# Dividing two vector-engine pairs around the first Fourier transform of a fused attention and two-MLP kernel

## The chip, the cores and the metric

The kernel runs on one core of a Trainium2 chip. The metric is the device time of one execution in microseconds (us), lower is better. The engines are TensorE (PE in the profile; PEld is its weight loading), VectorE (DVE), ScalarE (ACT), GpSimd (POOL) and SyncE (SP, which here only issues transfers). They run side by side and wait for each other on semaphores.

## The reference

Everything is float32. Attention has batch 4, 8 heads, 576 tokens and head width 64; only the 32 largest scores of a row are kept:

```python
scores = q @ k.T / sqrt(64)
kth = np.partition(scores, -32, axis=-1)[..., -32:-31]
attn = softmax(np.where(scores >= kth, scores, -1e9)) ; x = attn @ v      # x: (4, 576, 512)
mixed = real(fft(fft(x, axis=1), axis=2)) ; u = x + mixed                 # first block
u = u + relu(layernorm(u) @ w_ch1) @ w_ch2                                # 512 -> 2048 -> 512
out = u + relu(layernorm(u) * g_ln @ v_ch1) @ v_ch2                       # second block, own weights
```

## The kernel before

**Tiles and slots.** The scores are cut into 144 tiles of 128 rows by 576 columns (NT = 36 for each batch). The loop of each engine goes over "slots" s; in slot s, TensorE transposes the probabilities of tile s (`probs_T`, L684), makes the scores of tile s+4 (`scores`, L636/L642), multiplies the probabilities of a finished pair of tiles with the values (`values`, L700/L706) and transposes the result back (`values_back`, L715). ScalarE empties PSUM behind it: `probs_out` (L927), `scores_out` (L886), `x_out`, `x_back` (L951, which puts the rows of x into U and counts s_x_sb), and it computes the exponentials (`exps`, L915 and L920).

**Pairs on VectorE.** `pair(n)` handles tiles 2n and 2n+1. It has four rounds; each takes the 8 largest of both tiles (L1140, twice) and, except in the last, strikes them out (L1146, twice). Then a masking instruction for each tile (L1153) makes the final probabilities. Pair 17 is the last one of batch 0; pair 18 (tiles 36, 37) and pair 19 (tiles 38, 39) are the two at the "first seam".

**The later scores.** The scores of the last 72 tiles are made early, two tiles at a time: `scores_ahead(e)` (L663/L669) for e = 0 to 35 on TensorE into all four PSUM banks called Big, in slot e+1; `scores_aside(e)` (L897) on ScalarE copies them out in slot e+2, and `store_aside(e)` (L901) sends them to HBM. Each `scores_ahead` waits for the copy of the one before.

**The first seam.** When batch 0's attention is done, VectorE divides its rows by the sums of the softmax and forms sums and differences of mirrored rows and columns (`normal_x`, `pair_x`, `fold_x`, L1162 to L1206). From that TensorE makes the two-dimensional transform in ten "pieces" (`dft_piece`; 0 to 3 at L779/L786 along the tokens, 4 to 9 at L791/L796 along the width), which ScalarE copies out (`piece_out`, L958). They are made in slot SEAM = 37 and use the banks of Big, so the first waits for the copy of the last scores ahead (s_ah_sb) as well as for the folds (s_fold). `combine(0, j)` on VectorE (L1217 to L1228) adds pieces 4+2j and 5+2j to U, `own_stats` takes the layer norm's statistics (L1232, L1236), `normalise` (L1258) scales two blocks of rows, TensorE transposes them (`un_T`, L811), ScalarE and VectorE split them into a high and a low part (L976 and `first_low`, L1264), and the first MLP can start.

**The burst.** In slot START[0] = 39 seven units of the MLP (`mlp1` L735, `mlp2` L752) are made at once on TensorE; from then on there is one unit (at times two) in every slot.

The order on VectorE before: pair 18, then `normal_x(0)`, `pair_x(0)`, `fold_x(0)`; pair 19; then `combined(0, 0)` (combine and statistics), `combine(0, 1)`, the two `normalise(0, j)`, `own_stats(0, 1)`, the two `first_low(j)`, `combined(0, 2)`; pair 20.

Of the kernel before, what the change touches and what calls it, by code (L numbers as in the profile page):

```python
# [14 lines left out]
NT = NHP * TPP  # L15
# [22 lines left out]
WFS = 3  # L38
AHEAD = NT
ASIDE = 4  # L40
KEPT = TILES - 2 * AHEAD
SIDE = (B // 2) * NHP

# [2 lines left out]
BURST = 7  # L46
GROUPS = len(ORDER)
NUNITS = GROUPS * KF
SEAM = NT + 1
FIRST = NT + 3  # L50
SCORED = {4: FIRST + 1, 5: FIRST + 2}
DOUBLE = (45, 52, 59, 66, 71, 82, 87, 96, 101, 105, 111, 121, 126, 132, 138)
# [14 lines left out]
def slot_of(n):  # L67

    return SLOT_OF[n]
# [15 lines left out]
def closing_at(s):  # L85

    if s == START[0]:
        return []
    return [n for n in range(NUNITS) if slot_of(n) == s - 1][-1:]


def turn_slot(t):
# [46 lines left out]
def rstd_slot(p):  # L139

    if ready_pair(p) >= PAIRS:
        return START[p] - 10
    return SEAM + 1 if p == 0 else 2 * (ready_pair(p) - 1)


def width(c):
# [71 lines left out]
def build(nc, q, k, v, g2, w_raw, seq_t, wid_t, alt_t, w_low, sc_ahead, out):  # L218
# [4 lines left out]
    with ctx:  # L223
# [398 lines left out]
        def _(pe):  # L622
# [203 lines left out]
            for s in range(SLOTS):  # L826
                pieces = [(b, i) for b in range(B) for i in range(PIECES) if piece_slot(b, i) == s]
                units = units_at(s)
                if s < TILES:
                    if turns_at(s - 1):  # L830
                        pe.wait_ge(s_unT_sb, last_turn(s))
                    probs_T(s)
                    if s + RING < KEPT and s not in SCORED.values():
                        if last_piece(s) > last_piece(s - 1) > 0 or last_piece(s) == PIECES and s == SEAM + 1:
                            pe.wait_ge(s_pc_sb, last_piece(s))
                        scores(s + RING)
                for n in second_at(s - 1):
                    mlp2(n - 1)
                if s == START[0]:
                    for t in turns_at(s):  # L840
                        un_T(t)
                if s != START[0]:
                    for n in units:
                        if n not in second_at(s):
                            mlp1(n)
                    for t in turns_at(s):
                        un_T(t)
                if s != SEAM and pieces:
                    dft_piece(*pieces[0])
                if s < TILES:  # L850
                    values(s)
                for n in closing_at(s):
                    mlp2(n)
                if s != SEAM and pieces:
                    dft_piece(*pieces[1])
                if s < TILES:
                    values_back(s)
                for n in second_at(s):
                    mlp1(n)
                if 0 < s <= AHEAD:  # L860
                    scores_ahead(s - 1)
                if s == SEAM:
                    pe.wait_ge(s_tab, 48)
                    for b, i in pieces:
                        dft_piece(b, i)
                if s == START[0]:
                    for n in units:
                        mlp1(n)
                        if n > 0:
                            mlp2(n - 1)  # L870
                        if n in SCORED:
                            scores(SCORED[n] + RING)

        @block.scalar
        def _(act):
# [163 lines left out]
            for s in range(SLOTS):  # L1039
                pieces = [(b, i) for b in range(B) for i in range(PIECES) if piece_slot(b, i) == s]  # L1040
                if s < TILES:
                    probs_out(s)
                    if s == START[0]:
                        for t in turns_at(s):
                            un_out(t)
                    if 0 <= s - 2 < AHEAD:
                        scores_aside(s - 2)
                    if s + RING < KEPT:
                        if s not in SCORED.values():
                            scores_out(s + RING)  # L1050
                    elif s % 2 == 0 and s + RING < TILES:
                        scores_in((s + RING) // 2)
                    if s % 2 == 0 and s < 2 * KF:
                        weights_high(s + 1)
                    if 0 <= s - 2 < AHEAD:
                        store_aside(s - 2)
                    if s % 2 == 0 and s + 2 < TILES and s not in (START[0] - 3, START[0] - 1, START[0] + 1) and not late_exps(s):
                        exps(s + 2)
                        exps(s + 3)
                    if s % 2 == 1 and late_exps(s - 1):  # L1060
                        exps(s + 1)
                        exps(s + 2)
                if s != START[0]:
                    for n in units_at(s):
                        if n in second_at(s):
                            continue
                        relu_out(n)
                        if n >= UP:
                            w2_high(n)
                    for t in turns_at(s):  # L1070
                        un_out(t)
                if s != SEAM and pieces:
                    piece_out(*pieces[0])
                if s < TILES:
                    x_out(s)
                if s != START[0]:
                    for n in units_at(s):
                        if n not in second_at(s):
                            highs(n)
                for n in closing_at(s):  # L1080
                    if n % KF == KF - 1 and n < NUNITS - 1:
                        y_out(n // KF)
                if s != SEAM and pieces:
                    piece_out(*pieces[1])
                if s < TILES:
                    x_back(s)
                for n in second_at(s):
                    relu_out(n)
                    highs(n)
                for p in range(GROUPS):  # L1090
                    for j in range(SIZE[p]):
                        if scaled_by_act(p) and s == scale_slot(p, j):
                            normalise(p, j)
                if s % 2 == 1 and s + 1 < 2 * KF:
                    weights_high(s + 1)
                if s == SEAM:
                    exps(s + 1)
                    exps(s + 2)
                    for b, i in pieces:
                        piece_out(b, i)  # L1100
                        if i == 0:
                            high_1(0)
                        if i == 1:
                            high_2(0)
                            high_1(1)
                        if i == 2:
                            high_2(1)
                        if i == 3:
                            high_1(2)
                if s == START[0]:  # L1110
                    for n in units_at(s):
                        relu_out(n)
                        if n > 0:
                            highs(n)
                        if n in (1, 5):
                            exps(s + n // 2 + 1)
                            exps(s + n // 2 + 2)
                        if n in SCORED:
                            scores_out(SCORED[n] + RING)
                for n in units_at(s):  # L1120
                    if UP <= n + 2 < NUNITS:
                        w1_high(n + 2)

        @block.vector
        def _(dve):
            def pair(n):
# [3 lines left out]
                for r in range(ROUNDS):  # L1130
# [12 lines left out]
                    for a, s in enumerate(tiles):  # L1143
                        dve.wait_ge(s_top, t0 + 2 * r + a + 1)
                        src = sc[:, s % RING, :] if r == 0 else wk[:, a, :]
                        nc.vector.match_replace(out=wk[:, a, :], in_to_replace=top[:, s % RING, r, :], in_values=src,  # L1146
                                                imm_value=STRUCK).then_inc(s_struck, 1)
                for a, s in enumerate(tiles):
                    dve.wait_ge(s_exp, s + 1)
                    dve.wait_ge(s_top, t0 + 2 * (ROUNDS - 1) + a + 1)  # L1150
# [94 lines left out]
            def combined(b, j):  # L1245
                combine(b, j)
                own_stats(b, j)
# [47 lines left out]
            dve.wait_ge(s_init, 2)  # L1295
            for n in range(PAIRS):
                pair(n)
                if n == NT // 2:
                    normal_x(0)
                    pair_x(0)  # L1300
                    fold_x(0)
                if n == NT // 2 + 1:
                    combined(0, 0)
                    combine(0, 1)
                    for j in range(SIZE[0]):
                        normalise(0, j)
                    own_stats(0, 1)
                    for j in range(SIZE[0]):
                        first_low(j)
                    combined(0, 2)  # L1310
# [76 lines left out]
```

## Time and profile before

| | |
|---|---|
| three executions | 1359.71, 1361.39, 1363.40 us; median 1361.39 |
| the profiled execution | 1362.1 us in all; its span from first to last instruction 1360.3 us |
| busy share of the span | PE 92%, DVE 81%, ACT 59%, POOL 26% |
| mean granted TensorE clock | 0.977 of full speed |

All rows are from the profiled execution and count from the start of its span. A busy share is an average over the kernel; what matters for this change is the stretch from about 205 to 315 us, around the first seam.

### The profile page before, as it was taken

To read this page: it belongs to the slowest core of one execution; us is meant where nothing else is said; L and a number is where in the kernel's file an instruction comes from. 1 tells how busy PE (TensorE), PEld (TensorE's weight loads), DVE (VectorE), ACT (ScalarE), POOL (GpSimd) and SP (SyncE) were. 2 spreads that over 40 slices of the span, in tenths; PEclk is the share of its full clock that TensorE was granted. 3 is DMA by queue.
4 is the path that set the end of the run, shared out by engine and by line. 5 is a ranking of instruction groups with operands and counts; after the bars stand their busy time and mean duration, and the time that the engine had idled before them with its cause. 6 is when DMAs were issued, how large, how long until landed. Compare 5 with 4: busy or idle time off the path is not lost.

```text
span 1360.3 us, 22775 instructions
## 1 busy us (share of the span) xinstructions
PE 1252.0 (92%) x7944; PEld 1024.3 (75%) x7944; DVE 1101.4 (81%) x2196; ACT 798.4 (59%) x1586; POOL 356.6 (26%) x327
## 2 busy tenths in 40 slices
PE   5776778999999899999988999999989999999999
PEld 3444444787777778788876888887679999999997
DVE  7999999899999989999999779975484454646453
ACT  4777765578777646776665557664353434343442
POOL 2444430122232431223335123333030111212110
PEclk9989978999999899999999999999999999999999
DMA  7899993567757757777885577753244343333342
GB/s 249 321 338 340 327 325 145 186 223 252 244 194 259 236 189 251 267 259 241 263 285 197 168 231 238 259 195 129 80 153 142 123 148 117 128 115 127 119 148 85
DMA packets 118259, 282.21 MB, mean 207 GB/s; under 512 B 29825, under 2 KB 29826, under 8 KB 118146
## 3 DMA queue, kind: packets, MB, share of 16 engines
q1 hardware_dynamic: 106386, 233.55, 51.7%
q10 hardware_dynamic: 10368, 42.47, 8.3%
q0 software_dynamic: 1392, 4.73, 1.1%
q8 instruction: 65, 1.06, 0.3%
q14 instruction: 48, 0.39, 0.1%
HBM read 237.44 MB, written 42.73 MB: 206 GB/s over the span
## 4 chain that ended last, share of the span: by engine, by line
PE 57%; DVE 36%; issue 5%; ACT 1%; POOL 1%; DMA 1%; SPq 0%; ACTq 0%; DVEq 0%
PE Big L752 23%; DVE top L1140 15%; PE Big L735 15%; DVE wk L1146 14%; PE Sp L735 7%; DVE ex L1153 3%; PE Tp L684 3%; PE Sp L779 2%; PE Tp L706 2%; PE Sp L791 1%; DVE st L1232 1%; PE Tp L811 1%; PE Big L779 1%; PE Sp L642 1%; PE Big L791 0%
## 5 line engine op out<-in xcount | busy, mean ns | idle before, releaser
L752 PE MATMUL Big<-wr,hh 128*128 128x512 f32 x1152 | 361.4, 395 | 0.0
L735 PE MATMUL Big<-uh,wr 128*128 128x256 f32 (+1 forms) x1400 | 320.9, 319 | 7.1 <-ACT hh L990 6.8
L1140 DVE MAX8 top<-wk 128x8 f32<-128x576 f32 x432 | 304.3, 745 | 0.0
L735 PEld LDWEIGHTS Big<-uh,wr 128*128 128x128 f32 x1400 | 236.5, 191 | 26.3 <-issue 16.5
L752 PEld LDWEIGHTS Big<-wr,hh 128*128 128x128 f32 x1152 | 217.6, 189 | 41.1
L752 PE MATMUL Big<-wr,hl 128*128 128x512 f32 x576 | 238.7, 414 | 4.8 <-DVE wr L1285 4.6
L512 POOL TENSOR_TENSOR hl<-hf,hh 128x256 fp32r<-128x256 f32 (+1 forms) x126 | 108.5, 861 | 452.5 <-ACT hh L990 452.5
L735 PE MATMUL Big<-ul,wr 128*128 128x256 f32 (+1 forms) x700 | 218.6, 312 | 0.0
L1146 DVE MATCH_REPLACE8 wk<-top,wk 128x576 f32<-128x576 f32 x288 | 211.4, 741 | 0.0
L684 PE MATMUL Tp<-ident,ex 128*128 128x128 f32 x720 | 117.1, 289 | 47.2 <-DVE ex L1153 38.3
L927 ACT ACTIVATE pT<-Tp 128x640 f32<-128x640 f32 x144 | 101.1, 702 | 88.1 <-PE Tp L684 87.9
L684 PEld LDWEIGHTS Tp<-ident,ex 128*128 128x128 f32 x720 | 86.5, 146 | 87.6 <-issue 50.8
L990 ACT ACTIVATE hh<-Big 128x384 fp32r<-128x384 f32 (+1 forms) x175 | 75.5, 432 | 118.1 <-PE Big L735 118.1
L1153 DVE SCALAR_TENSOR_TENSOR ex<-sc,top,ex 128x576 f32<-128x576 f32 x144 | 124.6, 902 | 18.8 <-ACT ex L920 18.7
L752 PEld LDWEIGHTS Big<-wr,hl 128*128 128x128 f32 x576 | 108.5, 188 | 34.8 <-issue 15.7
L735 PEld LDWEIGHTS Big<-ul,wr 128*128 128x128 f32 x700 | 133.5, 191 | 0.0
L1140 DVE MAX8 top<-sc 128x8 f32<-128x576 f32 x144 | 101.6, 746 | 16.6 <-ACT sc L886 9.5
L1146 DVE MATCH_REPLACE8 wk<-top,sc 128x576 f32<-128x576 f32 x144 | 105.7, 741 | 0.0
L920 ACT ACTIVATE ex<-sc,nmx 128x576 f32<-128x576 f32 x144 | 104.0, 769 | 2.3
L506 POOL TENSOR_TENSOR wr<-wf,wr 128x1024 fp32r<-128x1024 f32 x32 | 75.3, 2368 | 111.3 <-DVE top L1140 109.3
L989 ACT ACTIVATE hf<-Big 128x256 f32<-128x256 f32 (+1 forms) x126 | 52.2, 414 | 82.0 <-PE Big L735 82.0
L706 PE MATMUL Tp<-pT,vn 128*64 128x128 f32 x1280 | 87.9, 286 | 12.4 <-ACT pT L927 11.9
(136 smaller groups left out, 1832.1 us busy)
## 6 DMA issues: line engine op xcount, KB each, us to landing
wf<-in_weights SPq DMA_DIRECT2D x208, 512.0 KB, 3.6
wr<-w_low SPq DMA_DIRECT2D x252, 256.0 KB, 4.3
sc<-in_weights SPq DMA_DIRECT2D x48, 512.0 KB, 3.2
sc<-sc_ahead ACTq DMA_DIRECT2D x36, 576.0 KB, 5.6
w_low<-wr SPq DMA_DIRECT2D x32, 512.0 KB, 6.6
sc_ahead<-U ACTq DMA_DIRECT2D x18, 576.0 KB, 5.2
sc_ahead<-un ACTq DMA_DIRECT2D x9, 576.0 KB, 4.1
sc_ahead<-yb ACTq DMA_DIRECT2D x9, 576.0 KB, 6.5
```

The costliest lines, as they stand in the source:

```text
L506: pool.tensor_tensor(wr[:, r, :, 1, :], wf[:, j % WFS, :, :], wr[:, r, :, 0, :].bitcast(f32), ALU.subtract).then_inc(s_wlow, 1)
L512: pool.tensor_tensor(hl[:, n % 2, 0:w], hf[:, n % 2, 0:w], hh[:, n % 2, 0:w].bitcast(f32), ALU.subtract).then_inc(s_hl[0], 1)
L684: last = nc.tensor.transpose(Tp[:, c * P:(c + 1) * P], ex[:, s % RING, c * P:(c + 1) * P], ident[:, :])
L706: last = nc.tensor.matmul(OT[h * D:(h + 1) * D, :], vn[:, par, c, h, 0:D], pT[:, h, c * P:(c + 1) * P], start=(c == 0), stop=(c == C - 1))
L735: last = nc.tensor.matmul(hidden(n), a[:, kd * P:(kd + 1) * P], x[:, kd, 0:P * SIZE[p]], start=(kd == 0 and j == 0), stop=(kd == KD - 1 an ...
L752: last = nc.tensor.matmul(Ac[:, j, :], a[:, n % 2, j * P:(j + 1) * P], w, start=(f == 0 and m == 0), stop=(f == KF - 1 and m == 2))
L920: nc.scalar.activation(ex[:, s % RING, 0:S], sc[:, s % RING, :], ACT.Exp, bias=nmx[:, s % RING:s % RING + 1], scale=1.0 / np.sqrt(D)).then ...
L927: nc.scalar.activation(pT[:, s % 2, :], Tp[:, 0:C * P], ACT.Copy).then_inc(s_pT_sb, 1)
L990: nc.scalar.activation(hh[:, n % 2, 0:w], hidden(n), ACT.Relu).then_inc(s_h_sb, 1)
L1140: nc.vector.max(top[:, s % RING, r, :], src).then_inc(s_top, 1)
L1146: nc.vector.match_replace(out=wk[:, a, :], in_to_replace=top[:, s % RING, r, :], in_values=src, imm_value=STRUCK).then_inc(s_struck, 1)
L1153: nc.vector.scalar_tensor_tensor(out=ex[:, s % RING, 0:S], in0=sc[:, s % RING, :], scalar=top[:, s % RING, ROUNDS - 1, 7:8], in1=ex[:, s % ...
```

## The change

Three things move. On VectorE, `normal_x(0)`, `pair_x(0)` and `fold_x(0)` are issued inside pair 18, behind its second strike-out, and `combined(0, 0)` inside pair 19, behind its third; the two `normalise(0, j)` go ahead of `combine(0, 1)`. On TensorE and ScalarE the ten pieces move from slot 37 to slot 35, and so stand ahead of the transposes of tiles 36 and 37. So that Big is free there, `scores_ahead(0..32)` stay in slots 1 to 33, and 33, 34, 35 are made in slot 35 behind tile 35's values, ahead of the pieces; the copies and stores of 0 to 31 stay, the one of 32 goes to the end of slot 33, and those of 33, 34, 35 to the end of slot 35. The exponentials of tiles 38 and 39 follow the copy of piece 2.

```diff
+LAST = AHEAD - 1
-SEAM = NT + 1
+SEAM = NT - 1
...
+def made_at(s):
+    if s == LAST:
+        return [LAST - 2, LAST - 1, LAST]
+    return [s - 1] if 0 < s < LAST - 1 else []
+def taken_behind(s):
+    return {LAST - 2: [LAST - 3], LAST: [LAST - 2, LAST - 1, LAST]}.get(s, [])
...
-    return SEAM + 1 if p == 0 else 2 * (ready_pair(p) - 1)
+    return START[0] - 1 if p == 0 else 2 * (ready_pair(p) - 1)
...
-                        if last_piece(s) > last_piece(s - 1) > 0 or last_piece(s) == PIECES and s == SEAM + 1:
+                        if last_piece(s) > last_piece(s - 1) > 0 or last_piece(s) == PIECES and s == NT + 2:
...
-                if 0 < s <= AHEAD:
-                    scores_ahead(s - 1)
+                for e in made_at(s):
+                    scores_ahead(e)
...
-                    if 0 <= s - 2 < AHEAD:
+                    if 0 <= s - 2 < LAST - 3:
                         scores_aside(s - 2)
...
-                    if 0 <= s - 2 < AHEAD:
+                    if 0 <= s - 2 < LAST - 3:
                         store_aside(s - 2)
...
+                for e in taken_behind(s):
+                    scores_aside(e)
+                    store_aside(e)
                 if s == SEAM:
-                    exps(s + 1)
-                    exps(s + 2)
                     for b, i in pieces:
                         piece_out(b, i)
+                        if i == 2:
+                            exps(START[0] - 1)
+                            exps(START[0])
...
+                    if n == NT // 2 and r == 1:
+                        normal_x(0)
+                        pair_x(0)
+                        fold_x(0)
+                    if n == NT // 2 + 1 and r == ROUNDS - 2:
+                        combined(0, 0)
...
-                if n == NT // 2:
-                    normal_x(0)
-                    pair_x(0)
-                    fold_x(0)
                 if n == NT // 2 + 1:
-                    combined(0, 0)
-                    combine(0, 1)
                     for j in range(SIZE[0]):
                         normalise(0, j)
+                    combine(0, 1)
                     own_stats(0, 1)
```

## Rows read from the trace of the kernel before

**Rows 1.** The page: span and busy time of the engines.

```profile
span 1360.3 us, 22775 instructions
PE 1252.0 (92%) x7944; PEld 1024.3 (75%) x7944; DVE 1101.4 (81%) x2196; ACT 798.4 (59%) x1586; POOL 356.6 (26%) x327
```

**Rows 2.** Chain that ended last, 190 to 330 us: start, us, what.

```profile
218.37 1.12 PE Tp L684 x5
...
227.77 4.56 PE Big L779 x14
...
252.05 1.44 PE Big L735 x12
...
312.41 0.66 ACT sc L886
```

**Rows 3.** Timeline of VectorE: start, us, instruction, idle time before it.

```profile
207.76 1.42 DVE L1140 MAX8 top<-sc 128x8 f32<-128x576 f32 x2
...
213.31 1.42 DVE L1140 MAX8 top<-wk 128x8 f32<-128x576 f32 x2
...
218.87 0.18 DVE L1162 TENSOR_SCALAR den<-dsum 128x32 f32<-128x32 f32 x1
...
226.81 1.40 DVE L1140 MAX8 top<-sc 128x8 f32<-128x576 f32 x2
...
235.13 1.40 DVE L1140 MAX8 top<-wk 128x8 f32<-128x576 f32 x2
...
241.42 0.43 DVE L1217 TENSOR_TENSOR xf<-xs 128x257 f32<-128x257 f32 x1 [3.42 <-ACT xs L958]
...
244.96 0.40 DVE L1217 TENSOR_TENSOR xf<-xs 128x257 f32<-128x257 f32 x1
...
250.33 1.29 DVE L1264 TENSOR_TENSOR ul<-Big,uh 128x512 fp32r<-128x512 f32 x2 [0.86 <-ACT uh L976]
...
253.10 1.42 DVE L1140 MAX8 top<-sc 128x8 f32<-128x576 f32 x2
...
289.52 1.42 DVE L1140 MAX8 top<-sc 128x8 f32<-128x576 f32 x2 [2.53 <-ACT sc L886]
...
313.10 1.42 DVE L1140 MAX8 top<-sc 128x8 f32<-128x576 f32 x2 [0.78 <-ACT sc L886]
```

**Rows 4.** Timeline of TensorE: start, us, instruction, idle time before it.

```profile
214.55 1.24 PE L669 MATMUL Big<-U 64*128 64x288 f32 x8
218.37 1.10 PE L684 MATMUL Tp<-ident,ex 128*128 128x128 f32 x5 [2.58 <-DVE ex L1153]
...
221.29 2.29 PE L669 MATMUL Big<-U 64*128 64x288 f32 x8 [0.55 <-ACT un L897]
...
227.61 4.72 PE L779 MATMUL Big<-seq,xf 128*128 128x320 f32 x14
...
246.07 0.76 PE L684 MATMUL Tp<-ident,ex 128*128 128x128 f32 x5
...
249.01 1.09 PE L811 MATMUL Big<-ident,un 128*128 128x128 f32 x8
250.03 1.31 PE L706 MATMUL Tp<-pT,vn 128*64 128x128 f32 x20
```

**Rows 5.** Timeline of ScalarE: start, us, instruction, idle time before it.

```profile
212.38 1.13 ACT L897 ACTIVATE U<-Big 128x1152 f32<-128x1152 f32 x1
...
214.72 0.28 ACT L951 ACTIVATE U<-Tp 128x128 f32<-128x128 f32 x1 [0.48 <-PE Tp L715]
```

**Rows 6.** Windows of 2 us: length, busy PE, PEld, DVE, ACT, POOL, clock, DMA, GB/s.

```profile
216.00:218.00 2.00, 0.00 (x0) 0.00 (x0) 2.00 (x4) 0.00 (x0) 0.00 (x0) 1.00 0.00 0
...
222.00:224.00 2.00, 2.00 (x11) 1.10 (x8) 1.97 (x3) 0.00 (x0) 0.00 (x0) 0.50 0.73 295
224.00:226.00 2.00, 2.00 (x12) 1.19 (x13) 2.00 (x7) 1.12 (x2) 0.00 (x0) 0.65 0.00 0
...
248.00:250.00 2.00, 2.00 (x16) 1.31 (x14) 1.47 (x5) 1.22 (x3) 0.00 (x0) 1.00 0.03 8
```

## The prediction

> **What bounds the kernel now.** I read the page first: PE is busy for 92% of the span, DVE for 81% [rows 1], which says only that both come near to being the bound somewhere. So I then read the chain of what ended last, in order of time, around the first seam. It runs through VectorE up to the masks of pair 18, goes over to TensorE at 218.37 (the transposes of tile 36), passes through the pieces (227.77) and into the MLP burst at 252.05, and stays on TensorE until ScalarE's copy of scores at 312.41, which VectorE waits for [rows 2]. Between these two points the end is set by TensorE alone, so the number that matters is the start of the first MLP unit, 252.05. If it moves by some amount, the release at 312.41 moves by the same amount. I see nothing behind it that takes up a shift of a microsecond or two.
>
> The timeline of VectorE shows how near it is. From 253.10 to 313.10 it is idle for only 2.53 + 0.78 = 3.3 us [rows 3]. So a gain on TensorE passes through for at most about 3.3 us before VectorE would set the end, while a loss passes through in full. In the seam itself VectorE waits for 3.42 us (for piece 5) and 0.86 us (for the split rows) [rows 3]; these 4.3 us are what the change could appear to remove, but they lie off the chain, beside TensorE.
>
> TensorE itself sits idle for 2.58 us ahead of 218.37 and 0.55 us ahead of 221.29 [rows 4], and the windows show the clock at 1.00 at first, then 0.50 (1.2 GHz) and back to 1.00 in the course of 224 to 226 [rows 6]: the same scores ahead take 2.29 us there and 1.24 us before, a factor of 1.85 [rows 4].
>
> **The change step by step.** I follow the new order until the first MLP unit.
>
> *Rows of tile 35.* VectorE used to reach the scaling long after them; now it reaches it behind the second strike-out of pair 18. Pair 18 begins at 207.76 and its third round at 213.31 [rows 3]; so the scaling could start at 213.3. It needs ScalarE's last copy of tile 35's rows, which ends at 214.72 + 0.28 = 215.0 [rows 5]. With the copies of the scores ahead (1.13 us each [rows 5]) gone from slots 34 and 35, ScalarE reaches the chain copy of probabilities, values, turn back, copy sooner; the exponentials it also does there stay, and part of the time was spent waiting for TensorE, so I count 0.8 of the 1.13 us. The rows are there at 214.2, and VectorE waits for 0.9 us. Queued behind this wait are only pair 18's own later rounds.
>
> *Scaling and folds.* They take 226.81 - 218.87 = 7.94 us [rows 3], unchanged: folds done at 214.2 + 7.9 = 222.1.
>
> *The three score pairs.* TensorE makes 33 to 35 behind tile 35's values, with Big held until each copy is out, so they are serial: from about 213.8, three times 1.24 us of matmul [rows 4] and 1.13 us of copy [rows 5] with some 0.05 us at each handover end at about 221.1. If the clock falls on the way, as it did behind a similar wait, the matmuls take 2.29 us each. One of them (the likely case, the fall coming as before near 218.5) makes it 222.1, level with the folds; all three make it 224.3. I take 222.1 and keep 224.3 for a rival. The three stores leave within these 7 us; buffer un, which `normalise` needs, is stored from about 218.6 and needed at 244, far apart. The loads that SyncE issues behind the high parts of the weights come earlier with the pieces, so they hold nobody up.
>
> *The pieces.* Begin to end they take 246.07 - 227.61 = 18.46 us at full clock [rows 4]. Now they stand behind a wait: TensorE has some 3.7 us of work between 213.8 and 222.1. Before, a stretch with less work than usual was followed by 0.50, and the clock was back near 225.4 (the window from 224 reads 0.65), 4.1 us after the last idle time at 221.29 [rows 4, 6]. No row has a piece at the low clock. Bounds: nothing is lost if the clock is up at 222.1; if it is down for as long as 7 us, 7 x (1 - 1/1.85) = 3.2 us. I take 4.1 us at the low clock, so 4.1 x (1 - 1/1.85) = 1.9 us, since the pieces are gapless work like that of 221 to 225. The pieces end at 222.1 + 18.5 + 1.9 = 242.5, which is 3.6 us earlier than the 246.07 of before.
>
> The Trainium skill has a rule here, in "TensorE: Matmul & The Clock Gate", section "Why this matters for your kernels": idle gaps between bursts of matmuls drop the clock to half. By that rule the change is unwise, since it puts the longest block of TensorE's seam behind a wait; the trace agrees, with 0.50 behind the 2.58 us of idle time. Without the rule the sum would have no 1.9 in it and end below zero, with it the sum ends as below.
>
> *The transposes that come after.* Tiles 36 and 37 used to be done ahead of the pieces, in part while TensorE waited anyway; now they stand between the pieces and the burst, in addition to tiles 38 and 39. For 38 and 39, from the end of the pieces to the first MLP unit, it was 252.05 - 246.07 = 5.98 us [rows 2, 4]. For 36 and 37 there is no turning of normalised rows: from the first transposes to where L811 began, 249.01 - 246.07 = 2.94 us, then values, 1.3 us [rows 4], and the copy and transpose back, about 0.7 us: 4.95 us. Together 10.9 us, so the first MLP unit starts at 242.5 + 10.9 = 253.4. That is 1.4 us later than 252.05.
>
> So the sum on TensorE: the pieces 3.6 us earlier, the transposes of two tiles 4.95 us inserted: +1.4 us.
>
> *Is VectorE in time?* Rest of pair 18: 218.87 - 213.31 = 5.56 us, to 227.7. Three rounds of pair 19: 235.13 - 226.81 = 8.32 us, to 236.0. Piece 5 was ready for it 241.42 - 227.61 = 13.8 us after the first piece began, so now at 222.1 + 13.8 + 1.9 = 237.8: a wait of 1.8 us where there were 3.42. The combination and statistics, 244.96 - 241.42 = 3.54 us, to 241.3; rest of pair 19, about 2.9 us, to 244.2 [all rows 3]. The two `normalise` end near 245.1; TensorE turns these rows only at 242.5 + 4.95 + 2.94 = 250.4. So VectorE has 5 us to spare and does `combine(0, 1)` and the statistics in them (3.6 us, to 248.7), then waits some 3 us for the split rows. The wait of 3.42 us has not vanished, it has moved and shrunk by little: 1.8 + 3 us instead of 4.3. Pair 20 starts 1.32 + 1.2 + 1.5 us behind the turning, at about 254.5 where it was 253.10. The exponentials of 38 and 39 leave ScalarE near 234, before pair 19's masks need them (241.3), and the copy of piece 3 is not held up by them.
>
> **Sum.** The span becomes 1360.3 + 1.4 = 1361.7; with the 1.8 us around it (1362.1 for the profiled execution) 1363.5. The median of the three runs shown is 0.7 us below the profiled execution, so the median should be 1362.8 us.
>
> **The rivals.**
> - *Pieces at full clock.* If TensorE's work in 213 to 222 keeps the clock up, the 1.9 us are not lost: -0.5 us, 1360.9. For it: three score pairs lie in that time, where before there was a window with no matmul at all [rows 6]. Against it: they leave idle gaps of 1.2 us each.
> - *VectorE's waits are what counts.* If the 3.42 + 0.86 us of VectorE's idle time in the seam [rows 3] disappeared from the end, it would be -4.3 us, 1357.1, faster by 0.31%. Against it: the chain runs through TensorE from 218.37 to 312.41 [rows 2], and only 3.3 us are idle on VectorE behind it.
> - *The score pairs are late.* All three at 2.29 us: the pieces begin at 224.3, so 2.2 us more: +3.6 us, 1365.0.
> - *Slower for certain: the clock falls in the longer row of transposes.* Four tiles in a row of short work with copies between them, 10.9 us. At the low clock the transposes took 1.10 us and more against 0.76 [rows 4]; as a bound by 1.85, all of it low would cost 9 us, half of it 4.6 us: +6.0, 1367.4. It decides (above 4.1 us in all) from 2.7 us more than my sum, that is if some six of the eleven microseconds are low. Against it: in 248 to 250, the same kind of work, the clock read 1.00 [rows 6].
>
> **Chances and range.** A measurement of this kernel tells about 0.3% (4.1 us) from no change. Forecast (+1.4) 0.50; full clock (-0.5) 0.15; late score pairs (+3.6) 0.11; VectorE's waits 0.08; low clock in the transposes 0.08; something small that I don't name, either way, 0.08. Faster by over 0.3%: 0.08. Slower by over 0.3%: the last rival and a share of the late pairs, 0.11. Within: 0.81. The range leaves out VectorE's rival and the low clock in the transposes and takes in the bounds of the clock (0 to 3.2 us at the pieces, 2.2 us ahead of them) and the spread of the runs: 1359.0 to 1366.0.
>
> **What would show it.** In the profile after: the folds end near 222.1 with about 0.9 us of idle time ahead of the scaling; the first piece starts within 0.1 us of them or of the last copy of scores; the clock reads 0.50 there and is back some 4 us later; pieces end near 242.5; four tiles' transposes follow, and L735 starts near 253.4; VectorE shows 1.8 us ahead of L1217 and 3 us ahead of L1264. The prediction is wrong if the release of VectorE near 312 is no longer by TensorE, if the pieces start later than 224, or if the shift at 252 is not the shift of the end.

## The result

The changed kernel takes 1371.95 us in the median of six executions (1364.67 to 1376.4), the kernel before 1361.47 us beside it (1358.85 to 1363.4). The ratio is 1.0083, 95% interval 1.0066 to 1.0100: slower, by 0.8% or some 11 us. I had forecast 1362.8 us with a range up to 1366.0. Two things stand out: the size, and the spread, 11.7 us where the kernel before has 4.6. The profiled execution is one of the better ones, 1367.93 us with a span of 1366.1.

The page of the profile after, to be held against [rows 1]: the busy times are the same within 2.1 us, and the span is 5.8 us longer. No engine does more work; something waits or runs at another pace.

```profile
span 1366.1 us, 22775 instructions
PE 1254.1 (92%) x7944; PEld 1022.7 (75%) x7944; DVE 1100.5 (81%) x2196; ACT 799.8 (59%) x1586; POOL 357.2 (26%) x327
```

The chain that ended last in the profile after (start, us, what):

```profile
221.29 2.32 PE Big L682 x8
...
223.63 1.14 ACT yb L910
...
224.90 8.99 PE Big L792 x14
...
259.83 1.45 PE Big L748 x12
...
320.19 0.66 ACT sc L899
```

The first MLP unit starts at 259.83 where it was 252.05 [rows 2], 7.8 us later, and ScalarE's copy that releases VectorE comes at 320.19 where it was 312.41, again 7.8 us: the shift passes through in full, as argued. The first piece is released not by the folds, which end at 223.81, but by the copy of the last scores ahead (yb, L910). The first run of matmuls of the pieces, x14 in the profile, takes 8.99 us where it took 4.72 [rows 4]. (Each float32 matmul of the program stands as two in the profile: x14 are seven of them, the six of pieces 0 and 1 and the first of piece 2.)

VectorE's timeline after, for [rows 3]:

```profile
215.88 0.18 DVE L1185 TENSOR_SCALAR den<-dsum 128x32 f32<-128x32 f32 x1 [2.49 <-ACT U L964]
...
223.21 0.67 DVE L1229 TENSOR_TENSOR xf<-xs 128x510 f32<-128x510 f32 x1
...
243.99 0.43 DVE L1240 TENSOR_TENSOR xf<-xs 128x257 f32<-128x257 f32 x1 [6.21 <-ACT xs L971]
...
258.12 1.29 DVE L1287 TENSOR_TENSOR ul<-Big,uh 128x512 fp32r<-128x512 f32 x2 [3.27 <-ACT uh L989]
```

VectorE's idle time in the seam has grown from 4.3 us to 12.0 us (2.49 + 6.21 + 3.27). TensorE's timeline, for [rows 4]:

```profile
215.41 1.24 PE L682 MATMUL Big<-U 64*128 64x288 f32 x8
217.88 2.19 PE L682 MATMUL Big<-U 64*128 64x288 f32 x8 [1.23 <-ACT U L910]
221.29 2.29 PE L682 MATMUL Big<-U 64*128 64x288 f32 x8 [1.22 <-ACT un L910]
224.90 8.99 PE L792 MATMUL Big<-seq,xf 128*128 128x320 f32 x14 [1.32 <-ACT yb L910]
...
248.64 0.77 PE L697 MATMUL Tp<-ident,ex 128*128 128x128 f32 x5
...
256.79 1.09 PE L824 MATMUL Big<-ident,un 128*128 128x128 f32 x8
```

ScalarE's timeline, for [rows 5]: the copy of score pair 32 and its store, now at the end of slot 33, stand ahead of tile 34's probabilities, which begin at 210.01 (208.03 in the kernel before), and tile 35's rows end at 215.57 + 0.28 = 215.85 (215.0 before).

```profile
208.14 1.13 ACT L910 ACTIVATE U<-Big 128x1152 f32<-128x1152 f32 x1 [0.84 <-PE Big L682]
209.30 0.33 ACTq L914 DMA_DIRECT2D sc_ahead<-U  x1
210.01 0.70 ACT L940 ACTIVATE pT<-Tp 128x640 f32<-128x640 f32 x1 [0.74 <-ACT U L910]
...
215.57 0.28 ACT L964 ACTIVATE U<-Tp 128x128 f32<-128x128 f32 x1 [0.48 <-PE Tp L728]
```

And the windows after, for [rows 6] (the first number behind the POOL column is the granted clock): score pair 33 still runs at full speed (1.24 us), 34 and 35 run at 0.50 or nearly (2.19 and 2.29 us), and so do the pieces until somewhere in the third of them. The clock is back at 1.00 in the course of 232 to 236.

```profile
224.00:228.00 4.00, 3.10 (x5) 1.68 (x6) 4.00 (x9) 0.76 (x1) 0.00 (x0) 0.50 0.37 148
228.00:232.00 4.00, 4.00 (x8) 1.67 (x6) 4.00 (x10) 0.96 (x2) 0.00 (x0) 0.50 0.01 3
232.00:236.00 4.00, 4.00 (x9) 0.92 (x8) 4.00 (x9) 1.47 (x3) 0.00 (x0) 0.61 0.36 115
236.00:248.00 12.00, 11.08 (x40) 5.89 (x39) 5.72 (x14) 5.15 (x12) 0.20 (x2) 1.00 0.62 188
```

The shift of 7.8 us splits exactly: the pieces start 2.7 us earlier (224.90 against 227.61), last 5.3 us longer (224.90 to 248.64, 23.7 against 18.5), and from their end to the first MLP unit it takes 5.2 us longer (11.2 against 6.0). Of the 5.3 us, 0.4 are not the clock's: TensorE waits 0.92 us for the copy ahead of piece 4 where it waited 0.53. At the end of the span 5.8 us are left of the shift. A later seam has pieces too, and in the kernel before their first x6 run at the low clock behind a wait of 2.50 us (3.72 us, and 0.57 in the window 949 to 953); in the kernel after, at 956.37, they take 2.08 us behind a wait of 2.49, which gives back 1.6 of the missing 2.0 us. The rows of the kernel before:

```profile
949.00:953.00 4.00, 4.00 (x8) 1.90 (x9) 2.33 (x5) 0.33 (x1) 0.00 (x0) 0.57 0.46 143
```

```profile
948.91 3.72 PE L779 MATMUL Sp<-seq,xf 128*128 128x320 f32 x6 [2.50 <-DVE xf L1206]
```

### The profile page after: what moved, and what is told of

Its sections match the earlier page's. It is cut to its first block, busy times and chain, and to the rows that moved or that the text cites. A ratio compares the mean times of both kernels' runs of the same rounds, so it can differ in the third digit from the quotient of the medians.

```text
span 1366.1 us, 22775 instructions
## 1 busy us (share of the span) xinstructions
PE 1254.1 (92%) x7944; PEld 1022.7 (75%) x7944; DVE 1100.5 (81%) x2196; ACT 799.8 (59%) x1586; POOL 357.2 (26%) x327
## 4 chain that ended last, share of the span: by engine, by line
PE 57%; DVE 33%; issue 5%; POOL 2%; ACT 2%; DMA 1%; ACTq 0%; SPq 0%; DVEq 0%; POOLq 0%
PE Big L765 22%; PE Big L748 15%; DVE top L1157 14%; DVE wk L1163 13%; PE Sp L748 7%; DVE ex L1176 3%; PE Tp L697 2%; PE Sp L792 2%; PE Tp L719 2%; PE Sp L804 1%; PE Tp L824 1%; DVE st L1255 1%; PE Big L792 1%; PE Big L682 1%; DMA sc<-sc_ahead 0%
## 5 line engine op out<-in xcount | busy, mean ns | idle before, releaser
L1176 DVE SCALAR_TENSOR_TENSOR ex<-sc,top,ex 128x576 f32<-128x576 f32 x144 | 124.1, 899 | 18.5 <-ACT ex L933 18.3
```

Of the source, the lines that this page charges most:

```text
L1176: nc.vector.scalar_tensor_tensor(out=ex[:, s % RING, 0:S], in0=sc[:, s % RING, :], scalar=top[:, s % RING, ROUNDS - 1, 7:8], in1=ex[:, s % ...
```

## The experiments

My theory after the result: most of the loss, and all of the spread, is TensorE's clock, which falls in the waits around the score pairs behind tile 35 and stays at 0.50 in the pieces for a time that varies. Its rival: the structure (late rows, serial score pairs, two more tiles ahead of the burst) costs it all. Experiments 1 to 4, 5 to 8 and 9 to 11 each ran on one chip beside the kernel before, whose medians there were 1360.39, 1360.20 and 1360.39 us. One of its 22 executions beside the first group took 1366.8 us, so the kernel before has a rare long one too; the other 21 lie within 5.4 us. All ratios are to the kernel before of the same group; a ratio is not quite the quotient of the medians. Each profile is one execution, not always a typical one.

**1. The changed kernel again.** No edit.

> The changed kernel itself, to see what its spread is made of (1364.7 to 1376.4 us so far). Clock theory: the time follows how long the granted clock stays at 0.50 from about 218 us on; with the low stretch ending near 235 us as in the first profile about 1368 us, with one that lasts through all ten pieces up to 1376 us, with one that ends by 228 us about 1364 us. Rival, structure alone (late rows of tile 35, serial score pairs, two more tiles ahead of the burst): the time should not spread more than that of the kernel before, which is within 5 us.

1376.49 us (1370.44 to 1376.84, four executions; ratio 1.0101, 1.0071 to 1.0130). The profiled one took 1376.68 us, as expected for a low clock through nearly all pieces. TensorE's timeline and the windows of it:

```profile
213.13 2.40 PE L719 MATMUL Tp<-pT,vn 128*64 128x128 f32 x20 [1.24 <-ACT pT L940]
...
226.97 8.99 PE L792 MATMUL Big<-seq,xf 128*128 128x320 f32 x14 [1.32 <-ACT yb L910]
...
257.86 0.77 PE L697 MATMUL Tp<-ident,ex 128*128 128x128 f32 x5
```

```profile
212.00:216.00 4.00, 2.49 (x21) 2.10 (x21) 1.28 (x3) 1.89 (x4) 0.00 (x0) 0.61 0.00 0
...
228.00:248.00 20.00, 19.47 (x33) 7.27 (x31) 10.69 (x24) 5.87 (x12) 0.00 (x0) 0.50 0.34 110
...
252.00:256.00 4.00, 4.00 (x14) 2.17 (x12) 3.85 (x9) 0.82 (x3) 0.19 (x1) 0.77 0.00 0
```

The same program, and the clock falls earlier and is back only after 252. It is down before the first score pair: tile 35's values take 2.40 us at 213.13 where they took 1.31 in the first profile, behind waits of 1.29 and 1.24 us for ScalarE's copies of probabilities, which the first profile has as well. So the waits around the score pairs, which my theory names, are not the only ones behind which it falls. The pieces last from 226.97 to 257.86, 30.9 us; the first MLP unit starts at 269.05, which is 17.0 us behind the kernel before: -0.6 (start) + 12.4 (pieces) + 5.2 (transposes behind). Between the two profiles of this kernel the start of the pieces differs by 2.1 us, their duration by 7.2, and the transposes by nothing. So what separates these two executions is the clock, most of it in the pieces.

**2. TensorE kept at work.** Matmuls whose result nobody reads, into the bank of scores that is free in slot 35.

```diff
+            def keep_busy(k):
+                for _ in range(k):
+                    nc.tensor.matmul(Sp[:, 0, 0:SO], ident[:, :], seq[:, 0, 0, :], start=True, stop=True)
...
+                if s == SEAM:
+                    pe.wait_ge(s_tab, 48)
+                    pe.wait_ge(s_sc_sb, SEAM + RING + 1)
                 for e in made_at(s):
                     scores_ahead(e)
+                    if s == SEAM:
+                        keep_busy(7 if e == made_at(s)[-1] else 3)
...
```

The two waits ahead of the score pairs cost nothing here: in the profile score pair 33 follows tile 35's transpose back without idle time.

> The changed kernel with matmuls that compute nothing used (identity by a table, 128x320) on TensorE in slot 35 where it waits: three behind each of the first two score pairs, seven ahead of the pieces. Clock theory: the clock stays at 1.00 through the pieces, the spread falls to that of the kernel before, and the first MLP unit starts near 224 + 18.5 + 11 = 253.5 us instead of 259.8: about 1362 to 1363 us. Rival, structure alone: no better than the changed kernel, about 1372 us, or worse by the time that the added matmuls take.

1365.85 us (1364.37 to 1366.47, eleven executions; ratio 1.0033, 1.0022 to 1.0045). The median fell by 10.6 us against the first experiment, and the spread from 6.4 us (four executions) to 2.1 (eleven), by adding work.

```profile
222.50 4.04 PE L774 MATMUL Sp<-seq,ident 128*128 128x320 f32 x14
226.37 4.71 PE L796 MATMUL Big<-seq,xf 128*128 128x320 f32 x14
...
245.22 0.77 PE L697 MATMUL Tp<-ident,ex 128*128 128x128 f32 x5
```

```profile
216.00:226.00 10.00, 10.00 (x47) 6.19 (x44) 9.90 (x21) 3.39 (x3) 0.00 (x0) 1.00 0.44 178
226.00:245.00 19.00, 18.07 (x62) 8.74 (x61) 16.09 (x35) 7.68 (x17) 0.62 (x2) 1.00 0.46 143
```

The clock is 1.00 throughout, and the x14 take 4.71 us again. I had put in too many, so the pieces start at 226.37, 2.6 us behind the folds; that is most of the 3 us that it is above what I expected. The first MLP unit starts at 256.4, +4.4 us, and the time is up by 0.33%, 4.5 us.

**3. No scores behind tile 35.**

```diff
+EARLY = 31
-    if s == LAST:
-        return [LAST - 2, LAST - 1, LAST]
-    return [s - 1] if 0 < s < LAST - 1 else []
+    if s >= EARLY:
+        return {EARLY: [30, 31], EARLY + 1: [32, 33], EARLY + 2: [34], EARLY + 3: [35]}.get(s, [])
+    return [s - 1] if 0 < s else []
...
```

> The changed kernel with no scores behind tile 35: score pairs 30 to 35 are made in slots 31 to 34 (two in 31, two in 32), each copied out at the end of its slot. TensorE is then idle from tile 35's values until the folds. If the serial chain of three score pairs is what costs (structure), the pieces start with the folds, at 222 to 223 us, 2 us or more ahead of the 224.9 us of the changed kernel, and the time falls by that, to about 1370 us or less. Clock theory: the longer idle time ahead of the pieces keeps the clock at 0.50 at least as long, the pieces take 23 us or more, and the spread stays.

1371.71 us (1369.02 to 1372.51, four executions; ratio 1.0076, 1.0054 to 1.0099). It doesn't separate the two as meant: the crowded copies on ScalarE delayed tile 35's rows themselves (VectorE waits 7.13 us for them), so the folds end at 228.3 and the pieces start at 228.48, not at 222. What it does show is TensorE behind 8.5 us with no matmul: the clock is at 0.50 in all of 216 to 238, 9.5 us of them in the pieces, and it falls once more within them (0.57 in 246 to 250). The pieces last 25.8 us, as the clock theory had it; the spread of four executions, 3.5 us, is not larger than that of the kernel before, which it had not.

```profile
228.48 8.99 PE L793 MATMUL Big<-seq,xf 128*128 128x320 f32 x14 [8.51 <-issue]
```

```profile
228.00:238.00 10.00, 9.52 (x16) 4.04 (x17) 10.00 (x22) 2.43 (x5) 0.00 (x0) 0.50 0.01 2
```

**4. Only the second division.** The kernel before, with `combined(0, 0)` inside pair 19 and the two `normalise` ahead of `combine(0, 1)`.

```diff
+                    if n == NT // 2 + 1 and r == ROUNDS - 2:
+                        combined(0, 0)
...
-                    combined(0, 0)
-                    combine(0, 1)
                     for j in range(SIZE[0]):
                         normalise(0, j)
+                    combine(0, 1)
```

> The kernel before with only the second division: the first combination inside pair 19, the two scalings ahead of the second combination; pieces and scores ahead stay where they were. Theory: VectorE now waits about 6.3 us inside pair 19 for piece 5 where it waited 3.4 behind it, the masks of tiles 38 and 39 come at about 247.8 us instead of 238.0, TensorE waits for them less than 2 us, and the time is 0 to 2 us above the kernel before, nothing that can be measured. Rival: this division is what costs, and the time is near 1370 us.

1362.17 us (1360.18 to 1362.96, twelve executions; ratio 1.0008, 0.9997 to 1.0018): no difference that its interval shows. VectorE waits for piece 5 inside the pair, and TensorE waits 1.08 us for the masks behind it; the first MLP unit starts at 253.62, +1.6 us.

```profile
241.54 0.43 DVE L1219 TENSOR_TENSOR xf<-xs 128x257 f32<-128x257 f32 x1 [6.44 <-ACT xs L958]
```

```profile
247.35 0.74 PE L684 MATMUL Tp<-ident,ex 128*128 128x128 f32 x5 [1.08 <-DVE ex L1155]
```

**5. Fewer added matmuls.** As 2, with 2, 2 and 3 in place of 3, 3 and 7.

> As the second experiment, but two added matmuls behind each of the first two score pairs and three ahead of the pieces, so that the added work ends before the folds. In the second experiment the pieces began at 226.37 us, 2.5 us behind the folds. If the clock holds, they begin at 223.9, the first MLP unit starts near 253.9 us (1.9 us behind the kernel before), and the time is near 1362.5 us. If the clock falls for want of work, it goes back toward the changed kernel, 1366 us or more, with its spread.

1361.19 us (1360.02 to 1363.66, eleven executions; ratio 1.0006, 0.9997 to 1.0015). Seven matmuls of no use leave no loss that the interval shows, where the change had 1.0083.

```profile
220.44 1.88 PE L774 MATMUL Sp<-seq,ident 128*128 128x320 f32 x6
222.87 4.82 PE L796 MATMUL Big<-seq,xf 128*128 128x320 f32 x14 [0.54 <-DVE xf L1237]
```

The pieces are now released by the folds, last 18.95 us (to 241.82), and the first MLP unit starts at 253.01: +1.0 us. That is 0.9 us better than expected, since in this profile VectorE goes on with tile 35's rows at 214.81 and not at 215.88; why is said further down.

**6 and 7. A mended structure, with and without added matmuls.** Score pairs 0 to 33 made by slot 32, exponentials moved out of the way; 7 is the same without `keep_busy`.

```diff
+EARLY = 30
+    if s >= EARLY:
+        return {EARLY: [29, 30], EARLY + 1: [31], EARLY + 2: [32, 33], LAST: [34, 35]}.get(s, [])
+    return [s - 1] if 0 < s else []
...
-                    if s % 2 == 0 and s + 2 < TILES and s not in (START[0] - 3, START[0] - 1, START[0] + 1) and not late_exps(s):
+                    if s % 2 == 0 and s + 2 < TILES and s not in (SEAM - 1, START[0] - 3, START[0] - 1, START[0] + 1) and not late_exps(s):
...
                 if s == SEAM:
+                    exps(SEAM + 1)
+                    exps(SEAM + 2)
...
-                        if i == 2:
+                        if i == 6:
...
```

> The change with its structure mended: score pairs 0 to 33 are made by slot 32 (two in slots 30 and 32), only 34 and 35 behind tile 35; the exponentials of tiles 36 and 37 move behind tile 35's rows, those of 38 and 39 behind piece 6; two added matmuls behind score pair 34, seven ahead of the pieces. Tile 35's rows are there by 213.3 us, the folds done at 221.3, the first MLP unit at 221.3 + 18.5 + 11.2 = 251.0 us, 1 us ahead of the kernel before: 1359.5 us or so, no difference that can be measured. If something other than the rows, the clock and the order behind the pieces costs, it stays above 1362.

> The same without the added matmuls. Clock theory: TensorE has two score pairs in the 9 us between tile 35's values and the folds, so the clock is at 0.50 when the pieces begin, and it costs 5 to 14 us: 1365 to 1374 us, with a spread like that of the changed kernel. Rival (structure alone): like the sixth within 1 us.

With: 1364.57 us (1362.44 to 1365.51, eleven executions; ratio 1.0026, 1.0017 to 1.0034), 5 us above what I expected. Without: 1371.44 us (1365.91 to 1373.7, four executions; ratio 1.0071, 1.0044 to 1.0098). The miss of the sixth lies ahead of the seam: two score pairs in a slot hold back the copies of the attention scores, and VectorE, which sets the pace there, waits 0.45 + 2.64 us for them. Tile 35's rows are there at 218.5 us where I had 213.3, and the first MLP unit starts at 256.36 where I had 251.0.

```profile
211.05 1.42 DVE L1168 MAX8 top<-sc 128x8 f32<-128x576 f32 x2 [2.64 <-ACT sc L908]
```

The pair of them is the cleanest test of the clock, since only the added matmuls and their waits differ: 6.9 us between the medians, and the two intervals don't meet. In the seventh the pieces wait 4.87 us for the folds and run at 0.51 in 224 to 238, about 12 us of pieces; they last 24.2 us where the sixth has 18.6 at a clock of 1.00.

```profile
226.00 8.99 PE L793 MATMUL Big<-seq,xf 128*128 128x320 f32 x14 [4.87 <-DVE xf L1232]
```

**8. Added matmuls in the kernel before.** Four, in slot 35.

```diff
                     scores_ahead(s - 1)
+                if s == NT - 1:
+                    pe.wait_ge(s_tab, 48)
+                    pe.wait_ge(s_sc_sb, s + RING + 1)
+                    keep_busy(4)
```

> The kernel before with four added matmuls in slot 35, where TensorE waits 2.58 us for the masks of pair 18. Clock theory: the clock stays at 1.00 from 216 to 226 us, but the pieces can start only with the folds, at 226.9 instead of 227.6 us, so at most 0.7 us are gained: no difference that can be measured. This says whether added matmuls in themselves speed up this kernel elsewhere; if they do, by 3 us or more, the reading of the second experiment is weakened.

1358.93 us (1357.69 to 1360.69, eleven executions; ratio 0.9988, 0.9980 to 0.9997). The clock stays at 1.00 in 216 to 228, the pieces start with the folds at 226.88, and the first MLP unit at 251.39, -0.7 us. So at this place of the kernel before the low clock cost almost nothing: it lay in work that would have waited for the folds anyway. The ratio says 0.12% in all.

```profile
226.88 4.79 PE L783 MATMUL Big<-seq,xf 128*128 128x320 f32 x14 [0.98 <-issue]
```

**9. The fifth, with the exponentials out of the way.** Added matmuls 2, 2, 4; `exps` placed as in 6, scores as in the change.

> The fifth experiment (added matmuls that end before the folds, here 2, 2 and 4), and the exponentials out of ScalarE's way: those of tiles 36 and 37 behind the last copy of scores in slot 35 instead of ahead of tile 35's rows, those of 38 and 39 behind piece 6 instead of piece 2. Scores stay where the change put them. Tile 35's rows come 1.2 us or so sooner, the copy of piece 3 waits for nothing: first MLP unit near 251.5 us, where the fifth had 253.0, and the kernel before 252.05. Time near 1359.7 us, no difference that can be measured. If it stays at 1361 us or above, the exponentials were not in the way.

1359.69 us (1358.55 to 1362.9, twelve executions; ratio 0.9996, 0.9986 to 1.0006), the time expected, though the first MLP unit starts at 252.43 and not at 251.5: tile 35's rows come 1.3 us sooner than in the change (VectorE goes on at 214.61 instead of 215.88), and the wait ahead of piece 4 is 0.53 instead of 0.92 us.

```profile
222.68 4.82 PE L796 MATMUL Big<-seq,xf 128*128 128x320 f32 x14
```

**10 and 11. Which wait?** Added matmuls 2, 2, 0, and 0, 0, 3.

> Added matmuls only behind the first two score pairs (two each), none ahead of the pieces; tells which of the waits lets the clock fall. If the waits between the score pairs matter, the clock is at 1.00 at the first piece and the time is near 1362 us; if the wait ahead of the pieces matters, the clock is at 0.50 in the pieces and the time is 1365 us or more.

> Added matmuls only ahead of the pieces (three). If the waits between the score pairs alone let the clock fall, it is at 0.50 by then, the added matmuls run at half the clock and the time is 1365 us or more, with the spread of the changed kernel; otherwise near 1362 us.

Between the score pairs only: 1362.75 us (1361.72 to 1369.86; ratio 1.0022, 1.0008 to 1.0036); nine of ten executions below 1364.6 and one at 1369.86. Ahead of the pieces only: 1365.25 us (1360.53 to 1366.55; ratio 1.0023, 1.0011 to 1.0035), with seven of ten above 1363.5. Each takes away most of the loss, neither all of it, and the two ratios don't differ; by the medians they are 2.4 and 4.9 us above the kernel before, and the eleventh's median is the one that its expectation gives to the waits between the score pairs (1365 us or more). In the profile of the tenth the clock was low in 213 to 219, from tile 35's values on and so ahead of the score pairs, and back before the pieces. In that of the eleventh score pair 35 ran at the low clock (2.29 us at 218.38), the clock was at 1.00 when the pieces began, and it fell again within them (0.72 in 234 to 240), which no profile with matmuls in all three waits shows. These two profiles are among the faster of their ten executions (1361.78 and 1361.25 us), so what the slower ones did was not seen, and the question which wait matters has no single answer here.

```profile
219.00:244.00 25.00, 22.75 (x88) 11.30 (x86) 24.00 (x52) 10.37 (x21) 0.91 (x2) 1.00 0.52 180
```

```profile
223.00:234.00 11.00, 10.07 (x32) 4.15 (x31) 11.00 (x25) 5.63 (x12) 0.00 (x0) 1.00 0.38 137
234.00:240.00 6.00, 6.00 (x18) 3.87 (x17) 3.74 (x9) 1.23 (x4) 0.00 (x0) 0.72 0.90 273
```

## Why the prediction was wrong

By its own steps, against the first profile after and the one of experiment 1:

| step | predicted | measured |
|---|---|---|
| tile 35's rows there | 214.2 | 215.85; 216.8 |
| scaling and folds | 7.94 us | 7.93; 7.92 |
| last copy of scores ahead | 222.1 | 224.77; 226.8 |
| first piece | 222.1 | 224.90; 226.97 |
| pieces last | 20.4 us (1.9 lost) | 23.7 (5.3 lost); 30.9 (12.4 lost) |
| to the first MLP unit | 10.9 us | 11.2; 11.2 |
| first MLP unit | +1.4 us | +7.8; +17.0 |
| passes through to 312 | in full | in full |

The difference to my +1.4 us is thus 6.4 us in the first profile: the pieces start 2.8 us late, last 3.3 us longer than I gave them, and the transposes behind take 0.3 us more. In the second profile it is 15.6 us: 4.9, 10.5 and 0.3. My own sign of being wrong, pieces that start later than 224, is there too.

**The step that failed** is "I take 4.1 us at the low clock ... since the pieces are gapless work like that of 221 to 225", together with its upper bound: "if it is down for as long as 7 us, ... 3.2 us". The mechanism was in the prediction, with its place and its sign, and the term of 1.9 us measured 5.3 (4.9 of them the clock's) in one profile and 12.4 in the other. The clock stayed at 0.50 for some 10, 11 and 12 us of pieces (first profile, experiments 3 and 7) and for some 27 in experiment 1. I took the length of a stretch at the low clock from work of another kind (transposes and scores, 221 to 225) and gave its bound no reason from a row; the trace of before has a low stretch of 8 us or more around 172 to 180 that I had read and left out, though TensorE is not busy in all of it (one of its windows is below).

```profile
174.00:176.00 2.00, 2.00 (x9) 1.30 (x9) 2.00 (x6) 0.77 (x2) 0.10 (x1) 0.50 1.20 341
```

"No row has a piece at the low clock" holds for the rows that I showed, not for the trace: the pieces at 948.91 have it, and there it was back within some 4 us. So that row would have spoken for my 4.1 us; it was one draw of a length that varies.

Experiments 2, 5 and the pair 6 and 7 show the cause: with the same order of work and matmuls added in the waits, the clock stays up, and by the medians 10.6 us (2 against 1) and 6.9 us (6 against 7) are gone. What is left in experiment 5 is +1.0 us at the first MLP unit, and a ratio of 1.0006. My sum without the clock gave -0.5; the pieces start 0.8 us later than in it (222.87 against 222.1), last 0.5 longer, mostly for the longer wait ahead of piece 4, and the transposes take 0.3 more. I had said that the exponentials of tiles 38 and 39 don't hold up the copy of piece 3; experiment 9, which moves them, has the old wait of 0.53 us there.

**The rows of tile 35** came 0.85 us later than before, where I counted 0.8 us gained because a copy of scores goes from slot 34. I missed that it goes to the end of slot 33, directly ahead of tile 34's probabilities on ScalarE, with its store behind it. It is in the way there only when it comes late, and that is the clock once more, ahead of the seam: in the profile after, the clock is 0.50 in 198 to 204 and score pair 31 takes 4.10 us (3.54 in the kernel before); in experiment 11 it is 1.00 there, the pair takes 2.16 us, and with the order of the change as it was the scaling starts at 213.92, near my 214.2.

```profile
198.68 4.10 PE L676 MATMUL Big<-U 64*64 64x288 f32 x16 [1.13 <-ACT un L910]
```

```profile
198.59 2.16 PE L676 MATMUL Big<-U 64*64 64x288 f32 x16 [1.13 <-ACT un L918]
```

```profile
213.92 0.18 DVE L1193 TENSOR_SCALAR den<-dsum 128x32 f32<-128x32 f32 x1 [0.61 <-ACT U L972]
```

Experiment 5 has that pair at 2.16 us too. Experiment 9 has it at 4.10 us, as the profile after, so these two compare: two exponentials moved out of the path bring the rows 1.3 us sooner.

**The serial score pairs.** I let them begin at 213.8 and one of three run at the low clock. They began at 215.41, since the work ahead of them was as late as the rows; two ran at the low clock, in experiment 1 three. The last copy ends at 224.77 and not at 222.1, of which the late start is 1.6 us and the second low pair 1.0. Each late pair puts off the first piece, since that needs Big. The first piece thus came about as late as in my rival of +3.6 us, by a late start and one more low pair, beside the failed step and not in its place.

**What held:** the chain, and with it that VectorE's waits are off it: they grew by 7.7 us, and TensorE never waited for VectorE between the folds and the first MLP unit. The order behind the pieces, +5.2 us against +4.95 in the sum, free of the clock in every profile. The rival with the low clock in the transposes behind the pieces did not happen: 1.00 there in every profile, whatever had gone before. Experiment 4 bounds the second division: alone it puts the first MLP unit 1.6 us later, nothing that the time shows. In the changed kernel TensorE doesn't wait for the masks of tiles 38 and 39.

The Trainium skill, "TensorE: Matmul & The Clock Gate", section "Why this matters for your kernels", had the direction: gaps between bursts drop the clock to half. The same page says under "What's actually happening" that "the default state is throttled, and activity releases the throttle". Here the first is borne out in the profile after and experiment 2 (1.00 before the waits, 0.50 behind them, 1.00 again with the waits filled), behind waits of 1.2 to 1.3 us each; the second held only late, since TensorE was busy for 19.5 of the 20 us in 228 to 248 of experiment 1 and the clock stayed at 0.50.

**What stays open.** Why the pieces, once begun at the low clock, keep it for 10 us in one execution and 27 in the next, and whether it is their shape: no run gave the same wait other work behind it. The mean granted clock of an execution does not settle it either: the best of the six had 0.977 and the worst 0.959, but one of 1374.02 us had 0.973, as much as the profiled one of 1367.93. A version clearly better than both kernels was not found: experiment 8, the kernel before with four added matmuls, is 0.12% faster (interval 0.03 to 0.20%), experiment 9 equals the kernel before. Of the 1.3 us by which the median of experiment 8 is lower, its profile shows 0.7 in the seam; the rest is not explained.

## What to carry to other kernels

When a change puts a dense block of matmuls behind waits that TensorE didn't have there, the larger price can be the block at half the clock and not the wait, as here, and the length of the low stretch isn't bounded by what other work in the trace took to get the clock back: take the whole block as the upper bound. Cheap to try before anything else: a few matmuls of no use in the wait, just fewer than fill it. A spread that grows with a change is a reason to look at the clock: profile more than one execution and read the granted clock over the same stretch, since the mean of a whole execution did not settle it here.

## What the runs showed of the hardware that was not expected

Nearly gapless float32 matmuls (128x320, from 246.37 on 128x258) ran at 0.50 for at least 24 us (228 to 252 in experiment 1), after score pairs with waits of 1.23 us between them. The first x14 take 8.99 us there and 4.71 at full clock, a factor of 1.9. The clock can also fall within the pieces with no new wait longer than 0.93 us (experiment 11, 234 to 240). Similar pieces behind a similar wait (2.50 and 2.49 us, at 948.91 before and 956.37 after) ran at the low clock in one profile and at the full one in the other. And matmuls that nobody needs, 8 us of TensorE's time in experiment 2 and 4.6 in experiment 5, made the changed kernel faster.
